# Other block widths, and another order of columns for each quarter of a block

## The chip, the cores and the metric

The kernel runs on one core of a Trainium2 chip. The metric is the device time of one execution in microseconds. The engines are TensorE (PE, with its weight loads shown apart as PEld), VectorE (DVE), ScalarE (ACT), GpSimd (POOL) and SyncE (SP), whose queue issues nearly all DMAs.

## What is computed

Two sequences of 6080 tokens with 256 channels pass through a gated scan along time, and each resulting token through a layer of 2048 hidden units with ELU. All is float32.

```python
    sig = 1.0 / (1.0 + np.exp(-f_logit))
    f = lower_bound[None, None, :] + (1.0 - lower_bound[None, None, :]) * sig
    i = 1.0 - f
    for t in range(S):
        h = f[:, t] * h + i[:, t] * x[:, t]
        y[:, t] = h
...
    h = x @ w_in
    g = np.where(h > 0.0, h, alpha * (np.exp(np.minimum(h, 0.0)) - 1.0))
    return (g @ w_out).astype(np.float32)
```

## The kernel before

Channels lie on the 128 partitions, tokens along the free dimension. The 6080 tokens of both sequences are worked on together, in 12 blocks along time: block 0 has `SHORT` = 448 tokens, blocks 1 to 11 have `TILE` = 512. `width(j)` and `tokens(j)` give a block's width and its place in memory.

Every operand of a matmul is split into a rounded part (`_hi`) and a rest (`_lo`), and a product is three matmuls: hi by hi, lo by hi, hi by lo. The layer's input product is computed in blocks 1 to 11 by seven products (`P1` to `P7`) for each pair of units instead of eight; there are 8 pairs (`q`) in a block. The function `product` issues its three matmuls at lines 866 to 868. The output product is `second`, with its three matmuls at lines 896 to 898. So a pair has 21 + 24 matmuls and a block 360, each of as many columns as the block has tokens. Block 0 is computed plainly: 32 tiles of 6 + 6 matmuls, 384 in all, at lines 968 to 1004 (input) and 896 to 898 (output); 17 of them are 512 columns wide although the block has 448. Ahead stand 18 matmuls on zeros in bfloat16 (line 1010) that warm the engine up.

Between the two products each tile passes through ScalarE (line 466 Relu of the negative, line 472 Exp, line 480 rounding to `g_hi`), VectorE (line 719, the ELU) and GpSimd (line 336, the rest `g_lo`). Beside that run, one block ahead, the gates (422, 613), the weighing (620), the scan (628) and the splitting of its result (451, 656, 356). The order on each engine is written out by hand as a function `whole(j, par)` for each engine, with semaphores between them. Blocks 3 to 10 are a hardware loop of two blocks a pass on PE, ACT and DVE; POOL and SP loop in a similar way. PE's instructions do not depend on a block's number except in the semaphore values they wait for.

The matmuls neither read nor write their columns in plain order. All three, moving operand in and result out, go through one function, so that each column still lands where it belongs:

```python
LINE = 8
APART = 4
...
def in_order(columns):

    return columns.rearrange("p (b a c) -> p a b c", a=APART, c=LINE)
```

The 512 columns are taken in runs of 8 neighbours; one run of every four is taken, 16 in all, and that is done in 4 passes over the columns. The pattern of a 512-column matmul is so 4 x 16 x 8, of a 448-column one 4 x 14 x 8.

Of the kernel before, what the change touches and what calls it, by code (L numbers as in the profile page):

```python
# [1 line left out]

# [19 lines left out]
SHORT = SEQ - (BLOCKS - 1) * TILE  # L22
# [8 lines left out]
LINE = 8  # L31
APART = 4
# [23 lines left out]
def in_order(columns):  # L56

    return columns.rearrange("p (b a c) -> p a b c", a=APART, c=LINE)


def width(j):
    return SHORT if isinstance(j, int) and j == 0 else TILE


def tokens(j):
    return bass.ds(0 if isinstance(j, int) and j == 0 else TILE * j - (TILE - SHORT), width(j))

# [8 lines left out]
def low_count(j, product):  # L76

    return j if product in (P6, P7, P3) else j + 1


def gated_scan_elu_ffn(nc, first_gate, forget_logit, value, w_in, w_out, out):
    ctx = ExitStack()
    with ctx:
# [139 lines left out]
        def _(sp):  # L223
# [24 lines left out]
            def reload(j):  # L248

                sp.wait_ge(carry_ready, BATCH * j)  # L250
                sp.wait_ge(a_lo_ready[P1], j)
                sp.wait_ge(sum_ready[1], j - 1)
                sp.wait_ge(sum_ready[2], j - 1)
                load_x(j, 0, 0)
                load_x(j, 1, 0)
                sp.wait_ge(a_lo_ready[P2], j)
                sp.wait_ge(sum_ready[3], j - 1)
                load_x(j, 0, 1)
                sp.wait_ge(a_lo_ready[P5], j)
                load_gate(j, 0, 0)  # L260
                sp.wait_ge(a_lo_ready[P6], j - 1)
                load_gate(j, 0, 1)
                sp.wait_ge(a_lo_ready[P7], j - 1)
                load_gate(j, 1, 0)
                sp.wait_ge(a_lo_ready[P3], j - 1)
                load_gate(j, 1, 1)

            def reload_last(j):
                sp.wait_ge(a_lo_ready[P4], j)
                load_x(j, 1, 1)  # L270
# [35 lines left out]
            with sp.Fori(2, BLOCKS - 3) as j:  # L306
                reload_last(j + 1)
                store(j - 1)
                reload(j + 2)
# [12 lines left out]
        def _(pool):  # L322
# [17 lines left out]
            def combine(j, k):  # L340
# [6 lines left out]
                if k == 1:  # L347
                    pool.wait_ge(sum_ready[0], j)
# [61 lines left out]
            with nc.Fori(0, (BLOCKS - 4) // 2, engines=(mybir.EngineType.Pool,),  # L410
                         hint_back_edge=True) as i:
                whole(2 * i + 2, 0)
                whole(2 * i + 3, 1)
# [4 lines left out]
        def _(act):  # L418
# [24 lines left out]
            def split(j, par, product):  # L443
# [5 lines left out]
                else:  # L449
                    act.wait_ge(sum_ready[(P5, P6, P7, P3).index(product)], j)  # L450
# [146 lines left out]
            with nc.Fori(1, (BLOCKS - 2) // 2, engines=(mybir.EngineType.Activation,),  # L597
                         hint_back_edge=True) as i:
                whole(2 * i + 1, 1)
                whole(2 * i + 2, 0)  # L600
# [8 lines left out]
        def _(dve):  # L609
# [22 lines left out]
            def combine(j, k):  # L632
# [6 lines left out]
                if k == 1:  # L639
                    dve.wait_ge(sum_ready[0], j)  # L640
# [6 lines left out]
                if k == 3:  # L647
                    dve.wait_ge(sum_ready[1], j)
# [198 lines left out]
            with nc.Fori(1, (BLOCKS - 2) // 2, engines=(mybir.EngineType.DVE,),  # L847
                         hint_back_edge=True) as i:
                whole(2 * i + 1, 1)
                whole(2 * i + 2, 0)  # L850
# [8 lines left out]
        def _(pe):  # L859
            def product(j, par, q, k, bank, start=False):  # L860
# [3 lines left out]
                into = in_order(bank[:, 0:w])  # L864
                a_h, a_l = in_order(a_h[:, 0:w]), in_order(a_l[:, 0:w])
# [161 lines left out]
            for t in range(TILES * (PAIRS - 1) - 1, TILES * PAIRS):  # L1027
                for half in range(HALVES):
                    second(j, t, half)
# [33 lines left out]
```

## Time and profile before

| | us |
|---|---|
| time before, two runs | 961.75 and 1004.33, median 983.04 |
| the profiled execution | 962.05 |
| its span in the profile | 960.2 |
| PE busy | 954.3 (99%) |
| ACT busy | 790.1 (82%) |
| DVE busy | 722.3 (75%) |
| POOL busy | 628.8 (65%) |

The span is the time between the first and the last instruction of the profile; 1.85 us of the execution lie around it. The profiled execution agrees with the faster of the two runs. A matmul's start is a measured time; its end is modelled, so that busy times of neighbouring matmuls overlap, and the distance from start to start is what tells how fast the engine goes.

### The profile page before, as it was taken

To read this page: it belongs to the slowest core of one execution; us is meant where nothing else is said; L and a number is where in the kernel's file an instruction comes from. 1 tells how busy PE (TensorE), PEld (TensorE's weight loads), DVE (VectorE), ACT (ScalarE), POOL (GpSimd) and SP (SyncE) were. 2 spreads that over 40 slices of the span, in tenths; PEclk is the share of its full clock that TensorE was granted. 3 is DMA by queue.
4 is the path that set the end of the run, shared out by engine and by line. 5 is a ranking of instruction groups with operands and counts; after the bars stand their busy time and mean duration, and the time that the engine had idled before them with its cause. 6 is when DMAs were issued, how large, how long until landed. Compare 5 with 4: busy or idle time off the path is not lost.

```text
span 960.2 us, 15016 instructions
## 1 busy us (share of the span) xinstructions
PE 954.3 (99%) x4362; PEld 815.4 (85%) x4362; DVE 722.3 (75%) x916; ACT 790.1 (82%) x1424; POOL 628.8 (65%) x477
## 2 busy tenths in 40 slices
PE   9999999999999999999999999999999999999998
PEld 6999888888888888888888888888888888888887
DVE  6998876976886796697688679679768867966444
ACT  7989888878888888888888888888888788887775
POOL 2578796576667668557656755856775765676544
PEclk9999999999999999999999999999999999999999
DMA  7212012002101201100210210120021021001001
GB/s 273 68 33 95 0 34 66 34 1 78 55 1 55 77 1 44 55 33 1 75 55 0 66 66 0 45 66 20 23 65 44 0 76 55 0 0 46 1 1 45
DMA packets 23078, 42.02 MB, mean 44 GB/s; under 512 B 2560, under 2 KB 4096, under 8 KB 23040
## 3 DMA queue, kind: packets, MB, share of 16 engines
q1 hardware_dynamic: 22752, 41.10, 13.2%
q10 hardware_dynamic: 288, 0.46, 0.1%
q8 instruction: 18, 0.29, 0.1%
q14 instruction: 20, 0.16, 0.1%
HBM read 29.10 MB, written 12.45 MB: 43 GB/s over the span
## 4 chain that ended last, share of the span: by engine, by line
PE 96%; ACT 2%; DVE 1%; issue 1%; POOL 0%; ACTq 0%; POOLq 0%
PE acc L896 17%; PE acc L898 17%; PE acc L897 17%; PE h L868 14%; PE h L866 14%; PE h L867 14%; ACT e L472 1%; PE h L1010 1%; PE h L1002 1%; PE h L1004 1%; PE h L1003 1%; ACT e L466 1%; DVE x L628 0%; PE h L968 0%; ACT w_out_hi L505 0%
## 5 line engine op out<-in xcount | busy, mean ns | idle before, releaser
L336 POOL TENSOR_TENSOR g_lo<-e,g_hi 128x512 fp32r<-128x512 f32 (+1 forms) x384 | 516.4, 1355 | 325.5 <-ACT g_hi L480 324.0
L466 ACT ACTIVATE e<-h 128x512 f32<-128x512 f32 (+1 forms) x379 | 224.8, 593 | 124.6 <-PE h L868 90.3
L719 DVE SCALAR_TENSOR_TENSOR e<-e,h 128x512 f32<-128x512 f32 (+1 forms) x379 | 256.8, 678 | 70.2 <-ACT e L472 69.1
L896 PE MATMUL acc<-g_hi,w_out_hi 128*128 128x512 f32 (+1 forms) x768 | 291.1, 379 | 0.4 <-DVE w_out_lo L690 0.4
L898 PE MATMUL acc<-g_hi,w_out_lo 128*128 128x512 f32 (+1 forms) x768 | 291.0, 379 | 0.0
L897 PE MATMUL acc<-g_lo,w_out_hi 128*128 128x512 f32 (+1 forms) x768 | 290.9, 379 | 0.0
L472 ACT ACTIVATE e<-e 128x512 f32<-128x512 f32 (+1 forms) x384 | 241.3, 628 | 9.7 <-issue 1.2
L480 ACT CAST g_hi<-e 128x512 fp32r<-128x512 f32 (+1 forms) x384 | 232.1, 604 | 19.3 <-DVE e L719 19.3
L866 PE MATMUL h<-a_hi,w_in_hi 128*128 128x512 f32 x616 | 234.7, 381 | 0.0
L868 PE MATMUL h<-a_hi,w_in_lo 128*128 128x512 f32 x616 | 234.7, 381 | 0.0
L867 PE MATMUL h<-a_lo,w_in_hi 128*128 128x512 f32 x616 | 234.7, 381 | 0.0
L896 PEld LDWEIGHTS acc<-g_hi,w_out_hi 128*128 128x128 f32 x768 | 143.9, 187 | 24.3 <-DVE w_out_lo L690 0.8
L897 PEld LDWEIGHTS acc<-g_lo,w_out_hi 128*128 128x128 f32 x768 | 143.9, 187 | 23.5
L898 PEld LDWEIGHTS acc<-g_hi,w_out_lo 128*128 128x128 f32 x768 | 143.9, 187 | 23.4
L868 PEld LDWEIGHTS h<-a_hi,w_in_lo 128*128 128x128 f32 x616 | 115.4, 187 | 20.1
L867 PEld LDWEIGHTS h<-a_lo,w_in_hi 128*128 128x128 f32 x616 | 115.4, 187 | 20.0
L866 PEld LDWEIGHTS h<-a_hi,w_in_hi 128*128 128x128 f32 x616 | 115.4, 187 | 20.0
L713 DVE TENSOR_TENSOR h<-p,h 128x512 f32<-128x512 f32 x88 | 60.9, 692 | 68.2 <-PE h L868 67.9
L628 DVE TENSOR_TENSOR_SCAN x<-opening,carry,x 128x512 f32<-128x512 f32 (+1 forms) x48 | 101.6, 2116 | 0.1
L698 DVE COPY p<-h 128x512 f32<-128x512 f32 x88 | 59.7, 679 | 43.4 <-PE h L868 42.9
L705 DVE TENSOR_TENSOR h<-p,h 128x512 f32<-128x512 f32 x88 | 60.7, 690 | 32.1 <-PE h L868 31.9
L620 DVE SCALAR_TENSOR_TENSOR x<-opening,x 128x512 f32<-128x512 f32 (+1 forms) x48 | 56.1, 1169 | 0.1
(77 smaller groups left out, 556.0 us busy)
## 6 DMA issues: line engine op xcount, KB each, us to landing
opening<-forget_logit SPq DMA_DIRECT2D x44, 256.0 KB, 2.7
x<-value SPq DMA_DIRECT2D x44, 256.0 KB, 2.7
out<-out_sb SPq DMA_DIRECT2D x44, 256.0 KB, 2.0
w_in_raw<-w_in SPq DMA_DIRECT2D x8, 256.0 KB, 5.4
w_out_raw<-w_out SPq DMA_DIRECT2D x8, 256.0 KB, 6.5
out<-out_sb SPq DMA_DIRECT2D x4, 224.0 KB, 1.9
x<-value SPq DMA_DIRECT2D x3, 224.0 KB, 6.1
opening<-forget_logit SPq DMA_DIRECT2D x2, 224.0 KB, 6.3
```

Source lines behind the costliest of these rows:

```text
L336: nc.gpsimd.tensor_tensor(g_lo[:, t % RING, 0:w], e[:, t % TILES, 0:w], g_hi[:, t % RING, 0:w].bitcast(F32), ALU.subtract).then_inc(g_lo_r ...
L466: nc.scalar.activation(e[:, i, 0:w], bank_of(j, t)[:, 0:w], ACT.Relu, scale=-1.0).then_inc(r_ready, 1)
L472: nc.scalar.activation(e[:, t % TILES, 0:w], e[:, t % TILES, 0:w], ACT.Exp, scale=-1.0).then_inc(e_ready, 1)
L480: nc.scalar.copy(g_hi[:, t % RING, 0:w], e[:, t % TILES, 0:w]).then_inc(g_hi_ready, 1)
L628: nc.vector.tensor_tensor_scan(x[:, b, i, 0:w], gate[:, b, i, 0:w], x[:, b, i, 0:w], carry[:, b, i], ALU.mult, ALU.subtract).then_inc(scan ...
L719: nc.vector.scalar_tensor_tensor(e[:, t % TILES, 0:w], e[:, t % TILES, 0:w], -1.0, bank_of(j, t)[:, 0:w], ALU.add, ALU.max).then_inc(g_rea ...
L866: nc.tensor.matmul(into, hi, a_h, start=start, stop=False, skip_group_check=True)
L867: nc.tensor.matmul(into, hi, a_l, start=False, stop=False, skip_group_check=True)
L868: return nc.tensor.matmul(into, lo, a_h, start=False, stop=True, skip_group_check=True)
L896: nc.tensor.matmul(bank, hi, g_h, start=opens, stop=False)
L897: nc.tensor.matmul(bank, hi, g_l, start=False, stop=False)
L898: done = nc.tensor.matmul(bank, lo, g_h, start=False, stop=closes)
```

## The change

The blocks become 496 and 504 tokens wide, then 512 and 504 in turns: six blocks of 504, five of 512 and one of 496 instead of eleven of 512 and one of 448. Since a block in a hardware loop now has a width by its parity, `width`, `tokens` and the semaphore counts go by a small class `Later` that holds the loop's number and whether it is odd; SP's loop takes two blocks a pass.

`in_order` takes a style. None is plain order, and block 0 has it. A style is (kind, groups, run, down): runs of `run` neighbours (4, 8 or 12 columns); kind T takes every `groups`-th run in `groups` passes as before; kind N with more than one group takes, within a stretch of groups times run columns, the runs one after the other, and N with one group takes all runs in a row; `down` walks a dimension backwards (1 the outer, 2 the middle, 4 the columns within a run). `STYLES` holds four for each of block 1, block 2, the odd blocks of the loop, its even blocks, and the last block: one for each quarter, which is two pairs. What was written as style (T, 4, 8, 0) in every block stands now in a part of the even blocks alone.

```diff
-SHORT = SEQ - (BLOCKS - 1) * TILE
+WIDTHS = (496, 504) + (512, 504) * (BLOCKS // 2 - 1)
+SHORT = WIDTHS[0]
...
-LINE = 8
-APART = 4
+T, N = range(2)
+FIRST_STYLE = None
+STYLES = (((T, 3, 8, 0), (T, 7, 8, 0), (T, 9, 8, 0), (T, 21, 8, 0)),
+          ((T, 2, 8, 0), (T, 4, 8, 1), (T, 4, 8, 2), (N, 1, 8, 2)),
+          ((T, 3, 12, 0), (T, 3, 4, 0), (T, 7, 4, 0), (T, 9, 4, 0)),
+          ((T, 4, 8, 0), (T, 4, 8, 4), (T, 8, 8, 0), (N, 4, 4, 2)),
+          ((T, 6, 4, 0), (T, 2, 12, 0), (T, 6, 12, 0), (T, 21, 4, 0)))
...
-def in_order(columns):
-
-    return columns.rearrange("p (b a c) -> p a b c", a=APART, c=LINE)
+def in_order(columns, style):
+    if style is None:
+        return columns
+    kind, groups, run, down = style
+    if kind == T:
+        steps = columns.rearrange("p (b a c) -> p a b c", a=groups, c=run)
+    elif groups == 1:
+        steps = columns.rearrange("p (o b c) -> p o b c", o=1, c=run)
+    else:
+        steps = columns.rearrange("p (b a c) -> p b a c", a=groups, c=run)
+    if down % 2:
+        steps = steps[:, ::-1]
+    if down // 2 % 2:
+        steps = steps[:, :, ::-1]
+    return steps[:, :, :, ::-1] if down // 4 else steps
...
 def width(j):
-    return SHORT if isinstance(j, int) and j == 0 else TILE
+    return WIDTHS[3 if j.odd else 2] if isinstance(j, Later) else WIDTHS[j]
...
             def whole(j, par, styles, before):
...
-                        second(j, TILES * at + i, half)
+                        second(j, TILES * at + i, half, styles[q // 2])
                     else:
-                        second(j - 1, TILES * (PAIRS + at) + i, half)
+                        second(j - 1, TILES * (PAIRS + at) + i, half, before)
```

No instruction moves against another on PE; the shapes change. The start of PE's program, before and then after (`h` and `acc` are banks of PSUM; a shape is partitions, then the pattern of columns from the outside in):

```order
L1010 MATMUL h<-e 128x512 x18
L968 MATMUL h<-a_hi,w_in_hi 128x4x16x8 x4
L968 MATMUL acc<-a_hi,w_in_hi 128x4x16x8 x2
L979 MATMUL h<-a_hi,w_plain_lo_54 128x4x16x8 x2
L983 MATMUL h<-a_lo,w_in_hi 128x4x16x8
L975 MATMUL h<-a_lo,w_in_hi 128x4x14x8
L979 MATMUL h<-a_hi,w_plain_lo_54 128x4x14x8 x2
```

```order
L1057 MATMUL h<-e 128x512 x18
L1015 MATMUL h<-a_hi,w_in_hi 128x512 x4
L1015 MATMUL acc<-a_hi,w_in_hi 128x512 x2
L1026 MATMUL h<-a_hi,w_plain_lo_54 128x512 x2
L1030 MATMUL h<-a_lo,w_in_hi 128x512
L1022 MATMUL h<-a_lo,w_in_hi 128x496
L1026 MATMUL h<-a_hi,w_plain_lo_54 128x496 x2
```

The wide ones stay 512 columns wide and the others grow from 448 to 496, all in plain order. In the loop on PE, where an odd block passes from its first quarter to its second, before and after:

```order
L898 MATMUL acc<-g_hi,w_out_lo 128x4x16x8
L952 REGISTER_ALU
L866 MATMUL h<-a_hi,w_in_hi 128x4x16x8
L867 MATMUL h<-a_lo,w_in_hi 128x4x16x8
L868 MATMUL h<-a_hi,w_in_lo 128x4x16x8
L922 REGISTER_ALU
L866 MATMUL h<-a_hi,w_in_hi 128x4x16x8
```

```order
L945 MATMUL acc<-g_hi,w_out_lo 128x3x14x12
L999 REGISTER_ALU
L913 MATMUL h<-a_hi,w_in_hi 128x3x14x12
L914 MATMUL h<-a_lo,w_in_hi 128x3x14x12
L915 MATMUL h<-a_hi,w_in_lo 128x3x14x12
L969 REGISTER_ALU
L913 MATMUL h<-a_hi,w_in_hi 128x3x42x4
```

The same instructions stand in the same places; the pattern and the width are other ones.

## Rows read from the trace of the kernel before

**Rows 1.** The page: span, busy time by engine, and the granted clock in 40 slices.

```profile
span 960.2 us, 15016 instructions
...
PE 954.3 (99%) x4362; PEld 815.4 (85%) x4362; DVE 722.3 (75%) x916; ACT 790.1 (82%) x1424; POOL 628.8 (65%) x477
...
PEclk9999999999999999999999999999999999999999
```

**Rows 2.** Waits between 80 and 955 us: engine, line, releaser, total us, times, longest.

```profile
POOL g_lo L336 <- ACT g_hi L480: 291.6, 236, 3.3
ACT e L466 <- PE h L868: 90.3, 167, 1.0
DVE h L713 <- PE h L868: 67.9, 68, 2.0
```

**Rows 3.** Timeline of PE: start us, duration us; the same place one block apart.

```profile
200.00 0.38 PE L897 MATMUL acc<-g_lo,w_out_hi 128*128 128x512 f32 x1
...
279.20 0.38 PE L897 MATMUL acc<-g_lo,w_out_hi 128*128 128x512 f32 x1
```

**Rows 4.** Timeline of PE: first matmul of block 1 and the last of all.

```profile
79.80 0.38 PE L866 MATMUL h<-a_hi,w_in_hi 128*128 128x512 f32 x1
...
956.58 0.40 PE L898 MATMUL acc<-g_hi,w_out_lo 128*128 128x512 f32 x1
```

**Rows 5.** Timeline of PE: a stretch of 169 matmuls of 448 columns, first and last.

```profile
12.49 0.35 PE L975 MATMUL h<-a_lo,w_in_hi 128*128 128x448 f32 x1
...
45.16 0.38 PE L1004 MATMUL h<-a_hi,w_plain_lo 128*128 128x448 f32 x1
```

**Rows 6.** Timeline of PE: warm-up matmuls after 6.2 us, merged where they overlap.

```profile
6.89 0.81 PE L1010 MATMUL h<-e 128*128 128x512 bf16 x3
...
7.32 0.38 PE L1010 MATMUL h<-e 128*128 128x512 bf16 x1
```

**Rows 7.** Timeline, from the first data to the first real matmul.

```profile
4.64 1.04 ACT L422 ACTIVATE opening<-opening 128x448 f32<-128x448 f32 x2 [1.69 <-DMA opening<-first_gate]
...
5.33 0.51 DVE L613 TENSOR_SCALAR opening<-opening,slope,offset 128x448 f32<-128x448 f32 x1 [0.45 <-ACT opening L422]
...
5.95 0.63 DVE L620 SCALAR_TENSOR_TENSOR x<-opening,x 128x448 f32<-128x448 f32 x1
...
6.61 1.15 DVE L628 TENSOR_TENSOR_SCAN x<-opening,carry,x 128x448 f32<-128x448 f32 x1
...
7.79 0.56 ACT L441 CAST a_hi<-x 128x448 fp32r<-128x448 f32 x1 [0.65 <-DVE x L628]
...
8.46 0.48 PE L968 MATMUL h<-a_hi,w_in_hi 128*128 128x512 f32 x1 [0.76 <-issue]
```

**Rows 8.** Timeline of PE: the last of four pauses in block 0.

```profile
66.28 0.38 PE L898 MATMUL acc<-g_hi,w_out_lo 128*128 128x448 f32 x1
66.79 0.45 PE L1002 MATMUL h<-a_hi,w_in_hi 128*128 128x448 f32 x1
67.07 0.37 PE L1003 MATMUL h<-a_lo,w_in_hi 128*128 128x448 f32 x1
67.28 0.36 PE L1004 MATMUL h<-a_hi,w_plain_lo 128*128 128x448 f32 x1
```

**Rows 9.** Groups by line and shape: x count | busy us, mean ns | idle us before.

```profile
L719 DVE SCALAR_TENSOR_TENSOR e<-e,h 128x512 f32<-128x512 f32 x352 | 240.2, 682 | 62.0 <-ACT e L472 61.3
...
L472 ACT ACTIVATE e<-e 128x512 f32<-128x512 f32 x352 | 222.6, 632 | 9.7 <-issue 1.2
...
L472 ACT ACTIVATE e<-e 128x448 f32<-128x448 f32 x32 | 18.6, 582 | 0.0
...
L719 DVE SCALAR_TENSOR_TENSOR e<-e,h 128x448 f32<-128x448 f32 x27 | 16.7, 617 | 8.2 <-ACT e L472 7.8
```

**Rows 10.** Timeline, the last copies and stores.

```profile
956.34 1.36 DVE L734 COPY out_sb<-acc 128x512 f32<-128x512 f32 x2 [1.29 <-PE acc L898]
...
957.06 1.00 SPq L276 DMA_DIRECT2D out<-out_sb  x2
```

**Rows 11.** DMA issues: KB each, median us to landing.

```profile
opening<-forget_logit SPq DMA_DIRECT2D x44, 256.0 KB, 2.7
...
opening<-first_gate SPq DMA_DIRECT2D x1, 225.0 KB, 3.9
```

More of the change, by code:

```diff
@@ L1 @@
 from contextlib import ExitStack
+from dataclasses import dataclass
 import concourse.bass as bass
@@ L53, with __add__, __sub__, __rmul__ @@
 PLACE = ((P1, P2), (P5, P4))
-def in_order(columns):
-    return columns.rearrange("p (b a c) -> p a b c", a=APART, c=LINE)
+def in_order(columns, style):
[13 more added lines that the diff above has]
+    return steps[:, :, :, ::-1] if down // 4 else steps
+@dataclass(frozen=True)
+class Later:
+    number: object
+    odd: bool
+    def __add__(self, k):
+        return Later(self.number + k, self.odd != bool(k % 2))
+    def __sub__(self, k):
+        return Later(self.number - k, self.odd != bool(k % 2))
+    def __rmul__(self, k):
+        return k * self.number
 def width(j):
-    return SHORT if isinstance(j, int) and j == 0 else TILE
+    return WIDTHS[3 if j.odd else 2] if isinstance(j, Later) else WIDTHS[j]
 def tokens(j):
-    return bass.ds(0 if isinstance(j, int) and j == 0 else TILE * j - (TILE - SHORT), width(j))
+    if not isinstance(j, Later):
+        return bass.ds(sum(WIDTHS[:j]), width(j))
+    known = 3 if j.odd else 2
+    step = (WIDTHS[2] + WIDTHS[3]) // 2
+    return bass.ds(step * j.number + (sum(WIDTHS[:known]) - step * known), width(j))
+def count(j):
+    return j.number if isinstance(j, Later) else j
 def split_count(j, product):
@@ L305, in _ @@
             reload(3)
[L306 to L309, printed above, removed]
+            reload_last(3)
+            store(1)
+            reload(4)
+            with sp.Fori(1, (BLOCKS - 4) // 2) as i:
+                for j in (Later(2 * i + 1, True), Later(2 * i + 2, False)):
+                    reload_last(j + 1)
+                    store(j - 1)
+                    reload(j + 2)
             reload_last(BLOCKS - 2)
@@ L859, in _, with product @@
         def _(pe):
-            def product(j, par, q, k, bank, start=False):
+            def product(j, par, q, k, bank, style, start=False):
                 w = width(j)
@@ L868, in product, with second @@
                 return nc.tensor.matmul(into, lo, a_h, start=False, stop=True, skip_group_check=True)
-            def second(j, t, half):
+            def second(j, t, half, style):
                 w = width(j)
@@ L902, in second, with whole @@
                     done.then_inc(acc_half, 1)
-            def whole(j, par):
+            def whole(j, par, styles, before):
                 def m(q, back, i, half):
@@ L922, in whole @@
                         pe.wait_ge(g_ready, TILES * (n - 2) + C21 + 1)
-                    product(j, par, q, P1, trunk(q), start=True).then_inc(p1_done, 1)
+                    product(j, par, q, P1, trunk(q), styles[q // 2], start=True).then_inc(p1_done, 1)
                     if q == 0:
@@ L926, in whole @@
                     pe.wait_ge(g_ready, TILES * (n - 1) + C12 + 1)
-                    product(j, par, q, P5, h[:, 2], start=True).then_inc(p5_done, 1)
+                    product(j, par, q, P5, h[:, 2], styles[q // 2], start=True).then_inc(p5_done, 1)
                     m(q, 2, C21, 0)
@@ L996, in first_product @@
                     hi, lo = plain_weights(unit, half)
-                    a_h, a_l = [in_order(part[:, 0:SHORT]) for part in a_parts(0, PLACE[b][half])]
+                    a_h, a_l = [in_order(part[:, 0:SHORT], FIRST_STYLE) for part in a_parts(0, PLACE[b][half])]
                     if t == TILES * PAIRS - 2 and half == 0:
-                        nc.tensor.matmul(in_order(h[:, 3]), hi, in_order(a_parts(0, P5)[0]), start=True, stop=False)
+                        nc.tensor.matmul(in_order(h[:, 3], FIRST_STYLE), hi, in_order(a_parts(0, P5)[0], FIRST_STYLE), start=True, stop=False)
                     else:
```

88 lines of the change are left out of this document (44 added, 44 removed).

## The prediction

> **What bounds the kernel now.** I read the page first [rows 1]: PE is busy 954.3 of 960.2 us, the next engine, ACT, 790.1, and the granted clock is in the top tenth in all 40 slices, the 2.4 GHz level of its two. Then the waits from 80 to 955 us [rows 2]: no row there has PE as the one that waits. Every other engine waits for PE or for an engine that does: ACT 90.3 us for line 868, DVE 67.9 us. So from block 1 on only PE's own rate counts, and the reader should look at the distance from start to start.
>
> From line 897 at 200.00 us to the same line 360 matmuls later it is 79.20 us, so 220.0 ns for each [rows 3]. From the first matmul of block 1 at 79.80 us to the last at 956.58 us [rows 4] there are 3989 steps, 30 of them still of block 0's 448 columns: 3959 x 0.2200 + 30 x 0.1933 = 876.8 us, and 876.78 us is what the rows say. PE does not lose one wait in 877 us. In block 0, 169 matmuls of 448 columns take 45.16 - 12.49 = 32.67 us, 193.3 ns each [rows 5].
>
> Two widths give a line: (220.0 - 193.3) / 64 = 0.417 ns per column, which is one column per cycle at 2.4 GHz, and what is left is 220.0 - 213.3 = 6.7 ns at 512 columns and 193.3 - 186.7 = 6.7 ns at 448. **So a matmul costs its columns plus 6.7 ns, 16 cycles**, whatever its operands are and whatever the other engines do. The only matmuls in plain order are the warm-up's. Three that follow each other start over 0.43 us [rows 6], 216 ns each, 4 ns less than the 220, but they read bfloat16 and load no float32 weights. The trace can't say whether the 4 ns are the order's or the type's. That is the open price of this change.
>
> **The widths.** With the constant of 6.7 ns, 504 columns cost 216.7 ns and 496 cost 213.3 ns. Six blocks of 360 matmuls go from 220.0 to 216.7: 2160 x -3.33 = -7.2 us. Five stay at 512. In block 0 the 17 wide matmuls stay, and 384 - 17 = 367 go from 193.3 to 213.3: +7.3 us. The sum is +0.1 us, since block 0 has 384 matmuls for a column and the others 360.
>
> **The start.** The chain to the first real matmul grows by 48 columns at each link: tanh, the gate (0.51 us), the weighing (0.63), the scan (1.15) and the rounding (0.56) [rows 7]. Exp takes 632 ns at 512 and 582 at 448 columns, the ELU 682 and 617 [rows 9], so 0.8 and 1.0 ns per column, some 40 and 50 ns for 48 columns; the scan by its own length 1.15 x 48 / 448 = 0.12 us. Together 0.3 us, and the first gate's transfer, 3.9 us for 225 KB [rows 11], adds up to 0.4 us if all of it goes by size and nothing if it is latency; a 256 KB load later lands in 2.7, so I take 0.1. The second scan and the rest of the second half stand behind the first on DVE and hold the next links: +0.4 us in all for the start, bounds 0.2 and 1.0.
>
> **The pauses in block 0.** PE pauses four times there, the last time at 66.28 us: 0.51 us to the next start and 0.28 to the one after, and then 0.21 us from 67.07 to 67.28 where 0.193 is the pace [rows 8]. Some 26 matmuls follow the pauses at about 0.20 to 0.21 us. A matmul of 496 columns takes 0.213 us anyway and hides this: -0.3 us. The pauses themselves I leave as they are, bounds -0.5 and +0.5, since the other engines grow by 8 to 9% in this block and PE by 10%.
>
> **From block 1 on.** What could take PE's cover away? At 504 columns PE is 1.5% faster, and the others are 8 columns shorter: 6 to 8 ns of 632 and 682, some 1.1%. PE gains at most 0.4% of 79 us = 0.3 us per block on them, and they wait for PE tens of times [rows 2]. Nothing. SP's loop is another one, but its loads land in 2.7 us [rows 11], and they are issued a block of 79 us ahead. Rows of 2016 instead of 2048 bytes change nothing that PE waits for. PE issues the same instructions in the same places, so no queue is lengthened.
>
> **The tail.** After the last matmul's start come two copies, 1.36 us, and the last stores [rows 10]: 8 columns less, -0.05 us.
>
> **The order of columns.** 3930 matmuls of blocks 1 to 11 have a pattern of runs. I take zero for each, because the nearest rows are those of the old pattern at two widths: 56 runs and 64 runs cost the same 6.7 ns, so a run costs nothing that can be seen. Block 0 in plain order I also take at zero; its lower bound is the warm-up's 216 ns: 384 x -4.0 = -1.5 us. The ends for all the others are in the rivals.
>
> The Trainium skill speaks against this change: "PSUM — Partial Sum Buffer", Specifications (TRN2), says of its 8-byte lines that any non-contiguous access pattern slows matmuls significantly, and "SBUF — State Buffer", Specifications (TRN2), that a 16-byte line wants at least two hits. By the trace the old pattern of 64 separate runs slows a matmul by at most 4 ns of 220 [rows 3, 6]; every new run is 4 columns or longer, thus fills whole lines, and the sum by that reading stays where it is.
>
> **The sum.** +7.3 - 7.2 + 0.4 - 0.3 - 0.05 = +0.2 us on the profiled execution's 962.05: **962.3 us**. It lies at the faster of the two runs shown, 961.75; the median of 983.04 is the mean of that and of 1004.33, which no row of the profile explains. I predict the level of the profiled execution; a measured median can hold a run like the second.
>
> **Rivals.**
>
> 1. *Each pass over the columns costs.* The 4 ns above the warm-up's pace could be those of the four passes, 1.0 ns each, and the rows don't exclude it, since both widths have four. The new styles make 1 to 9 passes, but 21 in 240 matmuls and 32 in the 510 of (N, 4, 4, 2). Over the 3930 matmuls they are 23,070 passes more than four each: +23.1 us, with block 0 in plain order -1.5 us: 984 us, 2.3% slower. It decides from 0.88 ns a pass up. For it: the only plain matmuls are the only faster ones. Against: the 4 ns can be all the type's.
>
> 2. *A short or a backward run is slow.* Patterns of 4 columns stand in 1890 matmuls and one in 360 walks backwards within the run, (T, 4, 8, 4). No row shows either. If the backward ones took two cycles a column, they would cost 360 x 213 ns = +77 us: 1039 us. By the smallest price, 4 ns spread over the 64 runs, 0.0625 ns for a run, the 108,600 additional runs cost +6.8 us, less 1.5 for block 0: 967.6 us. Against: the equal rest of 6.7 ns at 56 and 64 runs, where 8 runs at that price would be 0.5 ns.
>
> 3. *The orders save.* If none of the new orders has more than the warm-up's 2.7 ns, all 4344 matmuls gain 4.0 ns: -17.4 us, 945 us, 1.8% faster. This is the floor: a column per cycle stays. For it speaks only that some part of the 6.7 ns may be a meeting of one matmul's last lines with the next one's first.
>
> 4. *The second run's 1004 us come of the old order.* The profile that agrees with 961.75 shows full clock throughout, so the other 42 us are not in it. Should the old order bring them about and the new ones not, the time is the same 962, but 2.1% below the median of before. Nothing in the rows ties the two together.
>
> 5. *The change does not act*, the engine fetching columns in its own way whatever the pattern: the time is the forecast's, and only block 0's pace tells it.
>
> **Chances.** The forecast with its like (5, and all prices under a quarter of their ends) 0.62, the small price of 2 0.07, rival 3 in part or whole 0.05, rival 4 0.10, rival 1 0.10, the large price of 2 0.06. The range: the first three parts of the sum give 960 to 966; it goes up through 968 and 984, and on to 1003 since a run like the one at 1004.33 can enter a median; it goes down to 952, half of rival 3. That leaves out the large price of 2 and half of 3. About 2% is what a measurement of this kernel tells from no change. Faster by more: rival 4, 0.10. Slower by more: rival 1 and the large price, 0.16. Within: 0.74.
>
> **What the new profile would show.** Steps of 213.3 ns in block 0, 216.7 in the odd blocks and 220.0 in the even ones say the constant holds; 209 in block 0 says plain order saves 4 ns. If passes cost, the fourth quarter of the even blocks has steps of 248 ns and the last quarter of the last block 234. If backward runs are slow, the second quarter of the even blocks has them. The first `product` of block 1 should start at 79.8 + 7.3 - 0.6 (its 30 late matmuls of block 0) + 0.1 = 86.6 us. PE should still wait for nobody after that. The prediction is wrong if one quarter's step differs from the others of its width, or if PE waits for an engine from block 1 on.

## The result, and the profile after

The changed kernel takes 1048.38 us (1048.21 and 1048.56) against the kernel before's 983.04 (961.75 and 1004.33): 1.0895 times the time, 95% interval 1.0873 to 1.0917, against the faster of the two executions before; the other one has the time of a second, slower rate of the matmuls, which the experiments come to. It is slower by 87 us. The forecast was no change.

The page of the changed kernel, its span, its engines and its granted clock, beside [rows 1]:

```profile
span 1046.7 us, 14975 instructions
## 1 busy us (share of the span) xinstructions
PE 1040.4 (99%) x4362; PEld 822.9 (79%) x4362; DVE 725.9 (69%) x916; ACT 792.2 (76%) x1424; POOL 628.3 (60%) x477
...
PEclk9999999999999999999999999999999999999999
```

PE is as busy as before, 99%, the clock is at the 2.4 GHz level throughout, and DVE, ACT and POOL have the work they had. Only PE's own time has grown, by 86 us, for the same 4362 matmuls. The waits from 90 to 1040 us (engine, line, releaser, total us, times, longest) beside [rows 2]:

```profile
POOL g_lo L383 <- ACT g_hi L527: 377.7, 253, 5.1
ACT e L513 <- PE h L915: 171.7, 243, 1.7
DVE h L760 <- PE h L915: 94.2, 72, 3.0
```

Again everyone waits for PE and PE for nobody; ACT's wait has gone from 90.3 to 171.7 us. So each matmul is slower, and the timeline of PE says which. First and last of the 496-column matmuls ahead of block 1, the start of block 1, the start of the second and third quarter of an odd block of the loop, of the third and fourth quarter of the even block behind it, of the next block, and the last matmul (start us, duration us; the rows answer to [rows 3, 4]):

```profile
12.96 0.38 PE L1022 MATMUL h<-a_lo,w_in_hi 128*128 128x496 f32 x1
...
80.50 0.38 PE L945 MATMUL acc<-g_hi,w_out_lo 128*128 128x496 f32 x1
...
87.33 0.40 PE L913 MATMUL h<-a_hi,w_in_hi 128*128 128x504 f32 x1
...
276.53 0.39 PE L913 MATMUL h<-a_hi,w_in_hi 128*128 128x504 f32 x1
...
296.63 0.39 PE L913 MATMUL h<-a_hi,w_in_hi 128*128 128x504 f32 x1
...
380.51 0.39 PE L913 MATMUL h<-a_hi,w_in_hi 128*128 128x512 f32 x1
...
403.63 0.44 PE L913 MATMUL h<-a_hi,w_in_hi 128*128 128x512 f32 x1
...
427.63 0.40 PE L913 MATMUL h<-a_hi,w_in_hi 128*128 128x504 f32 x1
...
1042.76 0.40 PE L945 MATMUL acc<-g_hi,w_out_lo 128*128 128x504 f32 x1
```

Block 0, in plain order: from 12.96 to 80.50 us are 307 steps, 220.0 ns each, for 496 columns. From 276.53 to 296.63 is a quarter of 90 matmuls in the order (T, 3, 4, 0): 223.3 ns. From 380.51 to 403.63 is (T, 8, 8, 0): 23.12 us for 90, 256.9 ns. From 403.63 to 427.63 is (N, 4, 4, 2): 266.7 ns. From 87.33 to 1042.76 us the mean of 3989 steps is 239.5 ns, where it was 219.8. Most groups by order, over the whole trace (mean step in ns, and what it is above one column per 1/2.4 ns, in cycles of 2.4 GHz):

| order | columns | matmuls | ns | cycles above |
|---|---|---|---|---|
| plain | 496 | 367 | 220 | 32 |
| T 4 8 0, before | 512 | 3960 | 220.0 | 16 |
| T 3 4 0 | 504 | 360 | 223.3 | 32 |
| T 7 8 0 | 504 | 90 | 226.7 | 40 |
| T 4 8 0, after | 512 | 240 | 228.5 | 36 |
| T 3 12 0 | 504 | 240 | 230.8 | 50 |
| T 9 4 0 | 504 | 480 | 233.0 | 55 |
| T 7 4 0 | 504 | 360 | 233.3 | 56 |
| N 1 8 2 | 512 | 90 | 233.4 | 48 |
| T 4 8 4 | 512 | 360 | 235.7 | 54 |
| T 21 4 0 | 504 | 120 | 239.9 | 72 |
| T 21 8 0 | 504 | 120 | 241.7 | 76 |
| T 6 12 0 | 504 | 90 | 246.6 | 88 |
| T 8 8 0 | 512 | 360 | 256.9 | 105 |
| N 4 4 2 | 512 | 510 | 266.6 | 128 |
| T 6 4 0 | 504 | 60 | 286.5 | 183 |

Neither the number of runs nor that of passes sorts the table, nor does walking backwards. The old order itself has no longer one rate. At the start of each even block it stands in pieces of 6 or 9 matmuls between pieces of another order at 504 columns, and there its steps are 237 to 239 ns; the 33 matmuls from 352.01 us on, which nothing interrupts, have 220.7. The first such piece, six matmuls from line 913 on, and the next order behind it, 1.43 us for six:

```profile
338.62 0.39 PE L913 MATMUL h<-a_hi,w_in_hi 128*128 128x512 f32 x1
...
340.05 0.39 PE L943 MATMUL acc<-g_hi,w_out_hi 128*128 128x504 f32 x1
```

So a mean step belongs to an order in its surroundings. The weight loads are longer beside some of the slow matmuls. The groups of weight loads in the windows 352.1 to 358.5 us (old order), 380.6 to 403.5 (T 8 8 0) and 962.3 to 971.5 (T 6 4 0), x count, busy us and mean ns:

```profile
L943 PEld LDWEIGHTS acc<-g_hi,w_out_hi 128*128 128x128 f32 x6 | 1.1, 188 | 0.2
...
L944 PEld LDWEIGHTS acc<-g_lo,w_out_hi 128*128 128x128 f32 x16 | 3.1, 196 | 1.2
...
L943 PEld LDWEIGHTS acc<-g_hi,w_out_hi 128*128 128x128 f32 x6 | 1.2, 198 | 0.5
```

The loads are no measure of the matmuls: beside those of 266.6 ns they take 192 ns, and in the stretch of 256.9 ns those of line 945 take 188. Every matmul here brings its own 128 x 128 float32 weights, which are loaded beside the matmul ahead (PEld is busy for 822.9 us of the same span as PE's 1040.4). Two theories were made from this. **Theory R**: the reading of the moving operand out of SBUF meets the weight load that reads beside it, and which columns are read when decides how often. **Theory W**: the writing of the result into PSUM in an order sets the rate.

### The profile page after: what moved, and what is told of

Same layout as the page of the kernel before. It is cut to its first block, busy times and chain, and to the rows that moved or that the text cites. A ratio compares the mean times of both kernels' runs of the same rounds, so it can differ in the third digit from the quotient of the medians.

```text
span 1046.7 us, 14975 instructions
## 1 busy us (share of the span) xinstructions
PE 1040.4 (99%) x4362; PEld 822.9 (79%) x4362; DVE 725.9 (69%) x916; ACT 792.2 (76%) x1424; POOL 628.3 (60%) x477
## 4 chain that ended last, share of the span: by engine, by line
PE 99%; DVE 0%; DMA 0%; issue 0%; ACT 0%; DVEq 0%
PE acc L945 18%; PE acc L944 18%; PE acc L943 17%; PE h L915 14%; PE h L914 14%; PE h L913 14%; PE h L1050 1%; PE h L1051 1%; PE h L1049 1%; DMA opening<-first_gate 0%; PE h L1026 0%; DVE x L667 0%; DVE x L675 0%; PE acc L1051 0%; PE acc L1050 0%
## 5 line engine op out<-in xcount | busy, mean ns | idle before, releaser
L383 POOL TENSOR_TENSOR g_lo<-e,g_hi 128x504 fp32r<-128x504 f32 (+2 forms) x384 | 515.8, 1353 | 411.4 <-ACT g_hi L527 411.3
L513 ACT ACTIVATE e<-h 128x504 f32<-128x504 f32 (+2 forms) x379 | 225.0, 594 | 203.6 <-PE h L915 171.7
L945 PE MATMUL acc<-g_hi,w_out_lo 128*128 128x504 f32 (+2 forms) x768 | 309.9, 403 | 0.0
L944 PE MATMUL acc<-g_lo,w_out_hi 128*128 128x504 f32 (+2 forms) x768 | 308.8, 402 | 0.0
L943 PE MATMUL acc<-g_hi,w_out_hi 128*128 128x504 f32 (+2 forms) x768 | 308.2, 401 | 0.0
L766 DVE SCALAR_TENSOR_TENSOR e<-e,h 128x504 f32<-128x504 f32 (+2 forms) x379 | 256.5, 677 | 72.6 <-ACT e L519 72.2
L915 PE MATMUL h<-a_hi,w_in_lo 128*128 128x504 f32 (+1 forms) x616 | 248.6, 404 | 0.0
L519 ACT ACTIVATE e<-e 128x504 f32<-128x504 f32 (+2 forms) x384 | 241.4, 629 | 9.5 <-issue 1.1
L914 PE MATMUL h<-a_lo,w_in_hi 128*128 128x504 f32 (+1 forms) x616 | 247.7, 402 | 0.0
L913 PE MATMUL h<-a_hi,w_in_hi 128*128 128x504 f32 (+1 forms) x616 | 247.4, 402 | 0.0
L527 ACT CAST g_hi<-e 128x504 fp32r<-128x504 f32 (+2 forms) x384 | 232.2, 605 | 16.2 <-DVE e L766 15.6
```

The costliest lines, as they stand in the source:

```text
L383: nc.gpsimd.tensor_tensor(g_lo[:, t % RING, 0:w], e[:, t % TILES, 0:w], g_hi[:, t % RING, 0:w].bitcast(F32), ALU.subtract).then_inc(g_lo_r ...
L513: nc.scalar.activation(e[:, i, 0:w], bank_of(j, t)[:, 0:w], ACT.Relu, scale=-1.0).then_inc(r_ready, 1)
L519: nc.scalar.activation(e[:, t % TILES, 0:w], e[:, t % TILES, 0:w], ACT.Exp, scale=-1.0).then_inc(e_ready, 1)
L527: nc.scalar.copy(g_hi[:, t % RING, 0:w], e[:, t % TILES, 0:w]).then_inc(g_hi_ready, 1)
L766: nc.vector.scalar_tensor_tensor(e[:, t % TILES, 0:w], e[:, t % TILES, 0:w], -1.0, bank_of(j, t)[:, 0:w], ALU.add, ALU.max).then_inc(g_rea ...
L913: nc.tensor.matmul(into, hi, a_h, start=start, stop=False, skip_group_check=True)
```

## The experiments

Where no number of executions is given below, a kernel or scan was executed once.

**Orders with TensorE alone.** A kernel of matmuls only: 43 stretches of 60, every one with its own line, with the same layout of weights and moving operand as in the kernel (both at multiples of 512 bytes). The core of it:

```diff
+            def operands(name, w, read, write, shift, k):
+                at = P * (k % 8) + shift // 4
+                return (in_order(banks[:, (k // 3) % 8, 0:w], write), flat[:, at:at + P],
+                        in_order(moving[:, (k // 3) % 4, 0:w], read))
...
+            for k in range(EACH): last = nc.tensor.matmul(*operands('both_T4_512', 512, T4, T4, 0, k), **flags(k))
```

> TensorE alone: 43 stretches of 60 matmuls, each with the next weights loaded beside it, nothing else running and the results thrown away (the output is zeros). Both theories expect that the rates of the changed kernel come back here, with all other engines still: 220 ns in the old order at 512 columns, 227 ns in plain order at 512, 220 ns in plain order at 496, 257 for (T, 8, 8, 0), 267 for (N, 4, 4, 2), 286 for (T, 6, 4, 0). Theory R (the reading of the moving operand meets the weight load that runs beside it): reading in an order and writing plainly costs what both together cost, writing alone costs what plain order costs (227), a shift of the weights by 16 to 256 bytes changes the rate in the old order, and bfloat16, with half the bytes, is at 216 in every order. Theory W (the writing into PSUM sets the rate): the other way round, writing alone costs what both cost, reading alone 227, a shift of the weights changes nothing, and bfloat16 in the order (N, 4, 4, 2) is as slow as float32 in it. Rival 1 of the prediction, a price for each pass of the outer loop, expects 2 passes to be cheaper than 4 and 3 passes of 14 runs cheaper than 8 passes, and is nearly out already.

The timeline of PE, one row per stretch of 60 (start us, total us). The rows are: plain order at 512 columns; the old order at 512; the old order at 448; read in the old order and written plainly; read plainly and written in the old order; the start of the next; read in (N, 4, 4, 2) alone; written in (N, 4, 4, 2) alone; the start of the next; the old order with the weights shifted by 64 bytes; the start of the next; bfloat16 plain; bfloat16 in the old order; bfloat16 in (N, 4, 4, 2).

```profile
28.72 13.76 PE L149 MATMUL banks<-moving,weights 128*128 128x512 f32 x60
42.32 13.76 PE L151 MATMUL banks<-moving,weights 128*128 128x504 f32 x60
...
81.48 13.36 PE L157 MATMUL banks<-moving,weights 128*128 128x512 f32 x60
94.68 11.76 PE L159 MATMUL banks<-moving,weights 128*128 128x448 f32 x60
106.28 13.36 PE L161 MATMUL banks<-moving,weights 128*128 128x512 f32 x60
119.48 13.80 PE L163 MATMUL banks<-moving,weights 128*128 128x512 f32 x60
133.12 14.36 PE L165 MATMUL banks<-moving,weights 128*128 128x504 f32 x60
...
432.54 16.16 PE L207 MATMUL banks<-moving,weights 128*128 128x512 f32 x60
448.53 13.78 PE L209 MATMUL banks<-moving,weights 128*128 128x512 f32 x60
462.15 17.37 PE L211 MATMUL banks<-moving,weights 128*128 128x504 f32 x60
...
520.83 14.52 PE L219 MATMUL banks<-moving,weights 128*128 128x512 f32 x60
535.19 13.95 PE L221 MATMUL banks<-moving,weights 128*128 128x512 f32 x60
...
576.82 13.12 PE L227 MATMUL banks<-moving_b,weights_b 128*128 128x512 bf16 x60
589.78 13.11 PE L229 MATMUL banks<-moving_b,weights_b 128*128 128x512 bf16 x60
602.73 13.11 PE L231 MATMUL banks<-moving_b,weights_b 128*128 128x512 bf16 x60
```

Start to start over 60: plain 13.60 / 60 = 226.7 ns; the old order 13.20 / 60 = 220.0; reading in it alone 220.0, writing in it alone 227.3 with the first steps, 226.7 once it is steady. (N, 4, 4, 2) costs 266.5 when read and 227.0 when written. The old order at weights 64 bytes off costs 239.3. And bfloat16 runs at 215.8 to 216.0 ns in all three orders: that is what the warm-up's 216 ns [rows 6] were, the type's. The readings of theory R come in and those of theory W fail; only the shift by 256 bytes is no evidence, since its 230.8 ns turn out below to be a second rate of the old order. With all other engines still most of the changed kernel's rates come back within 1 ns, so those engines have no part in them. Five did not come exactly: (T, 8, 8, 0) had 241 ns instead of 257, (T, 21, 4, 0) 233.4 instead of 239.9, 496 columns in plain order 223.3 instead of 220.0, and (T, 3, 8, 0) and (T, 4, 8, 1) 236.6 and 236.3, each 3 ns above the kernel's.

**Plain order in the kernel before.**

```diff
-    return columns.rearrange("p (b a c) -> p a b c", a=APART, c=LINE)
+    return columns
```

> The kernel before with all columns in plain order. The changed kernel's block 0 in plain order takes 220.0 ns for 496 columns, 13.3 ns above one column per cycle, where the old order has 6.7. Both theories expect 13.3 ns on every matmul: 962.05 + 4344 x 6.67 ns = 991 us, the steps 226.7 ns at 512 columns and 200.0 at 448. The prediction as it stood expects 962 or, by the warm-up's pace, 945.

It took 989.51 us, the median of four executions, 1.0284 times (1.0262 to 1.0306), as the theories had it to 1.5 us; the old order is worth 28 us against plain order.

**One side at a time.** In the first kernel the moving operand is read in the old order and the result is written plainly, in the second the other way round. The two texts on record say it of each other's kernel; what ran is this, `apart` being the old order and `in_order` plain in the first, the names exchanged in the second:

```diff
                 into = in_order(bank[:, 0:w])
-                a_h, a_l = in_order(a_h[:, 0:w]), in_order(a_l[:, 0:w])
+                a_h, a_l = apart(a_h[:, 0:w]), apart(a_l[:, 0:w])
```

> The kernel before, with plain order for reading the moving operand, and the old order (T, 4, 8, 0) for writing the result alone; the columns of a result land in other places, so the output is not the reference's. Theory R: plain reading sets the rate, 991 us. Theory W: the old order of writing is what counts, 962 us.

> The kernel before, with the old order (T, 4, 8, 0) for reading the moving operand and plain order for writing the result; the columns of a result land in other places, so the output is not the reference's. Theory R: 962 us. Theory W: 991 us.

Read in the old order: 961.89 us. Written in it: 989.63. Read against the kernels themselves this is theory R, in both.

So as to have it once with a text that fits, and for the new orders, the same was done to the changed kernel, reading in its orders in one and writing in them in the other:

```diff
-                into = in_order(bank[:, 0:w], style)
+                into = bank[:, 0:w]
...
-                bank, g_h, g_l = in_order(bank, style), in_order(g_h, style), in_order(g_l, style)
+                bank, g_h, g_l = bank, in_order(g_h, style), in_order(g_l, style)
```

> The changed kernel with its orders for reading the moving operand, and plain order for writing the result; the columns of a result land in other places, so the output is not the reference's. Theory R: reading alone costs all of it, 1048 us. Theory W: plain writing, 998 us. (Of the two kernels before of this kind, the one called e2_read read in the old order and wrote plainly and e3_write read plainly and wrote in the old order, the other way round than their texts say; this one is described as it is.)

> The changed kernel with plain order for reading the moving operand and its new orders for writing the result; the columns of a result land in other places, so the output is not the reference's. Theory R: as with everything in plain order, 998.4 us. If writing costs anything of its own, more, up to 1048.

1048.70 us and 998.46 us. In the first, each order's mean step is that of the changed kernel to 0.1 ns. The writing of a result in any of these orders, all with runs of 4 columns or more, costs nothing that can be seen; the reading costs all.

**The widths alone.** The changed kernel with every style None:

```diff
-STYLES = (((T, 3, 8, 0), (T, 7, 8, 0), (T, 9, 8, 0), (T, 21, 8, 0)),
...
+STYLES = ((None,) * 4,) * 5
```

> The changed kernel's widths with all columns in plain order. By the rates in the traces so far, 226.7 ns at 512 and at 504 columns and 220.0 at 496: 3960 x 6.67 ns + 367 x 26.7 ns above the kernel before, so 962 + 26.4 + 9.8 = 998 us. By the sum of the prediction (16 cycles on every width) it would be 962. If the widths cost nothing against plain order at 448 and 512, it is 990.

998.40 us, against 989.51 for the old widths in plain order: the widths cost 8.9 us. In plain order 504 columns take 226.7 ns as 512 do, so the six narrower blocks give nothing back; and 448 columns took 202.7 ns, 496 take 220.0, so block 0 pays 367 x 17.3 ns = 6.4 us.

**More orders and distances.** The first scan's kernel with other cases, 36 matmuls in each.

> TensorE alone, 101 stretches of 36 matmuls (output zeros): many orders at 512 and 448 columns with weights and moving operand as they lie in the kernel, the old order and plain order with the weights shifted by 16 to 480 bytes. Theory R (reading the moving operand meets the weight load beside it in SBUF) expects the rate of one order to go up and down with the shift, between 216 and some 260 ns, and expects orders better than the old one's 220 ns to be possible down to bfloat16's 215.8. The rival (the pattern's own jumps cost, by their number and length) expects one rate per order whatever the shift, 220 for the old one and 227 for plain order; the first scan's five shifts of the old order already gave 227 to 240, so it is out unless those were after-effects of the stretch before.

No order at 512 columns beat 220.0 ns. The next was runs of 4 in 4 passes, 224.0; plain order and the orders that stay near it had 226.6 to 228.4, all others up to 278. Runs of 2 are another thing: rows are runs of 2 in 4 passes, then the old order with the weights 32 and 64 bytes off.

```profile
612.57 16.78 PE L293 MATMUL banks<-moving,weights 128*128 128x512 f32 x36
629.17 8.47 PE L295 MATMUL banks<-moving,weights 128*128 128x512 f32 x36
637.48 8.76 PE L297 MATMUL banks<-moving,weights 128*128 128x512 f32 x36
```

16.60 / 36 = 461 ns for a matmul. Here reading and writing both went by runs of 2, so which side costs it was not tested. The old order with the weights shifted by 32 to 480 bytes had 226.7 to 238.9 ns, and 220.0 at 256 bytes alone. But at no shift at all it had 230.6 here and 220.0 in the first scan, and in the first scan 230.8 at 256. So there are two rates. Plain order goes by the distance as well: 228.9 to 234.0 ns with the weights shifted by 16 to 448 bytes, but 227.2 at 256.

**Two rates for the old order.** 24 stretches of 48 in the old order, each after a pause of ScalarE's making:

```diff
+            pe.wait_ge(slept, 1)
             for k in range(EACH): last = nc.tensor.matmul(*operands('T4_0', 512, T4, T4, 0, k), **flags(k))
```

> TensorE alone (output zeros): 24 stretches of 48 matmuls in the old order at 512 columns, then 6 in plain order, 6 in (T, 8, 8, 0) and 4 of 448 columns in the old order, each stretch after a pause whose length grows by some ns from one to the next. If a stretch keeps the rate that it falls into at its start (as 496 columns in plain order had 220.0 ns in the changed kernel and 223.3 in the first scan), some of the 24 have another rate than 220 ns, perhaps around 230, which is what 1004 us for the kernel before would need on every matmul. If the rate goes by order and addresses alone, all 24 have 220.0 ns, and the 1004 us come from elsewhere.

Five of them on the timeline, alike in everything but the moment at which they begin:

```profile
97.71 11.34 PE L173 MATMUL banks<-moving,weights 128*128 128x512 f32 x48 [0.31 <-ACT pause L129]
109.37 11.34 PE L176 MATMUL banks<-moving,weights 128*128 128x512 f32 x48 [0.32 <-ACT pause L129]
121.03 10.84 PE L179 MATMUL banks<-moving,weights 128*128 128x512 f32 x48 [0.32 <-ACT pause L129]
132.19 11.34 PE L182 MATMUL banks<-moving,weights 128*128 128x512 f32 x48 [0.33 <-ACT pause L129]
143.86 11.34 PE L185 MATMUL banks<-moving,weights 128*128 128x512 f32 x48 [0.33 <-ACT pause L129]
```

Four of the 24 take 10.84 us, with steps of 219 and 221 ns from first to last. Twenty take 11.3 to 11.4, with steps of 227 to 237 ns, 230.7 in the mean. After their first steps none of these changes from one rate to the other. A rate is a pattern of steps that repeats: 219 and 221 ns in turns make 220.0, and 228, 229, 230, 230, 237 make 230.7. The old order at 448 columns has two as well, 193.3 ns in three stretches and 200.0 in the fourth. So has (T, 8, 8, 0), steps of 233 and 234 ns or of 246 to 277, and it can pass from one to the other: one of its six stretches was at 233 after four steps, one after 26 steps between 227 and 271, and four had not come to it within 48. The one in the first scan took about 28, which is why it had 241 ns and not 257. Plain order has one rate in six stretches.

Then in the kernel before, with one more wait on PE ahead of block 1:

```diff
                 second(0, TILES * PAIRS - LEAD, half)
+            pe.wait_ge(g_ready, TILES * PAIRS - 1)
             whole(1, 1)
```

> The kernel before with one more wait on TensorE ahead of block 1: it waits for the ELU of block 0's tile 30 (of 32), so that it stands for one to three microseconds and starts again at another moment. The last scan showed two rates for the old order at 512 columns, 220.0 ns in 4 of 24 stretches and 230.7 in 20, kept from the stretch's start to its end. If that holds in the kernel, where nothing stops TensorE from block 1 on, an execution takes either 963 to 965 us or 42 us more, 1005 to 1007, by chance or always the same one. If the rate goes by order and addresses alone, every execution takes 963 to 965.

Of its 11 executions one took 1004.66 us, one 965.23 and nine 961.4 to 961.9. Of the 13 of the kernel before on the same chip one took 1004.60, two 965.1 and 965.4 and ten 961.5 to 962.4. The wait cost nothing and changed nothing; the second time is the kernel's own. In the one execution with a trace PE did not even stop at it, so a start at another moment was not tested in the kernel. The executions at 965 us have no trace, and their 3 us stay open. The profiled execution was the one at 1004.66 us. The same line at the same place, 360 matmuls apart, beside [rows 3]:

```profile
200.18 0.40 PE L866 MATMUL h<-a_hi,w_in_hi 128*128 128x512 f32 x1
...
283.22 0.40 PE L866 MATMUL h<-a_hi,w_in_hi 128*128 128x512 f32 x1
```

83.04 / 360 = 230.7 ns, the second rate to the digit. It is so from 92 us to the end, for 3932 matmuls; 10.7 ns x 3960 = 42 us is what lies between 962 and 1004. By its time this is also the 1004.33 of the first table, of which no trace was kept. Full clock, no wait, the same matmuls.

It begins ahead of block 1 and of the added wait. In block 0 this execution comes back to 193.3 ns per matmul of 448 columns behind each of the first three pauses, as the kernel before does. Behind the fourth the kernel before is back at 193.3 after 16 uneven steps, and this one is at 200.0, the other rate of 448 columns: 18 steps in 3.60 us at the end of the block.

```profile
66.35 0.38 PE L898 MATMUL acc<-g_hi,w_out_lo 128*128 128x448 f32 x1
66.72 0.44 PE L1002 MATMUL h<-a_hi,w_in_hi 128*128 128x448 f32 x1
...
76.44 0.36 PE L1002 MATMUL h<-a_hi,w_in_hi 128*128 128x448 f32 x1
...
80.04 0.39 PE L866 MATMUL h<-a_hi,w_in_hi 128*128 128x512 f32 x1
```

The pause is 0.37 us from start to start here and 0.51 in [rows 8]. While widths alternate, up to 92 us, its 512-column steps lie anywhere from 219 to 238 ns; from about 94 us on the five steps of 230.7 ns repeat. That the length of the pause decides is not shown: it is one trace of each.

**Distance or place.** The moving operands 64 bytes further on, then all of SBUF's tiles 64 bytes further on, then the moving operands 256 bytes further on:

```diff
-        sb("room_of_edge", [P, P - EDGE])
+        sb("room_of_edge", [P, P - EDGE + 16])
...
-        sb("room_before", [P, -base % 512], mybir.dt.uint8)
+        sb("room_before", [P, -base % 512 + 64], mybir.dt.uint8)
...
-        sb("room_of_edge", [P, P - EDGE])
+        sb("room_of_edge", [P, P - EDGE + 64])
```

> The kernel before with all moving operands (and gates and x) 64 bytes further on in SBUF, the weights where they were. Theory R (the moving operand's reading meets the next weights' load, by the addresses of both): as weights shifted by -64 = 448 bytes in the scan, 229.9 ns at 512 columns, so 962 + 3960 x 9.9 ns and some more in block 0, about 1001 to 1005 us. Rival (the order's own jumps, addresses don't matter): 962.

> The kernel before with weights and moving operands both 64 bytes further on. If the distance between the two counts, 962 us (or 1004 by the second rate); if each one's own place counts, 1001 or more as with the moving operands alone.

> The kernel before with the moving operands 256 bytes further on and the weights where they were. Shifted by 64 bytes it took 988.5 us. The scans had the old order at 220.0 or 230.7 ns with the weights shifted by 256 bytes, as with no shift, and at neither with any other shift but one. If SBUF's lines come round again after 256 bytes: 962 us (or 1004 by the second rate). If only the same place within 512 bytes does: another time, 975 to 1010.

988.53, 961.81 and 961.96 us. The order is the same in all three and so is every instruction; what counts is the distance between weights and moving operand, and 256 bytes are as none. The 988.53 us are below the 1001 that the scan's 229.9 ns gave: in the kernel the steps were 231, 230 and 219 ns in turns, 226.7 in the mean. A distance has more than one rate, too, and a rate from a scan is not sure to be the kernel's.

**The weights' side.**

```diff
-                return (in_order(banks[:, (k // 3) % 8, 0:w], write), flat[:, at:at + P],
+                return (in_order(banks[:, (k // 3) % 8, 0:w], write), taken(k, at, step),
```

> TensorE alone (output zeros), two stretches of 36 matmuls for each pair of an order of the moving operand (18 of them) and a step between the weights' columns (1, 2 or 4 elements, weights interleaved with those of the next tiles). Theory R: the step changes the rate with the moving operand's order unchanged. A version faster than 220.0 ns would be worth a run in the kernel; down to bfloat16's 215.8 would be -18 us. If the moving operand's order alone makes the rate, the three steps have the same one.

The step changes the rate with the moving operand's order unchanged: plain order has 227.7 ns with adjacent weights, 233.3 with every second and 235 with every fourth; the old order 230, 231 and 238. The lowest of the 54 pairs was 223.5 ns once steady, runs of 4 in 4 passes with every second weight. No version faster than the kernel before was found, so none was run.

**Do the prices add up?** The changed kernel with the old order in the even blocks of the loop:

```diff
-          ((T, 4, 8, 0), (T, 4, 8, 4), (T, 8, 8, 0), (N, 4, 4, 2)),
+          ((T, 4, 8, 0), (T, 4, 8, 0), (T, 4, 8, 0), (T, 4, 8, 0)),
```

> The changed kernel with the old order (T, 4, 8, 0) in all four quarters of the loop's even blocks. If the price of an order is its own stretch's and adds up, it follows from the changed kernel's trace: 360 matmuls of (T, 8, 8, 0) from 256.9 to 220.0 ns, 510 of (N, 4, 4, 2) from 266.6 and 360 of (T, 4, 8, 4) from 236.0, together -42.8 us, 1006 us, since the first quarter of these blocks runs at 220.0 there; with the old order's second rate of 230.7 ns in all 1470 of them it is 1021. If the slow quarters are slow because orders change, or by something else than their order, less comes back.

1007.88 us, 2 us above the sum and far from 1021: these three orders in 1230 matmuls were worth 40.5 us. To about 2 us an order's price is its own stretch's. The expectation took 220.0 ns for the old order in these blocks; it has 222.2 over 1470 matmuls, because its pieces between other orders still take up to 239, and that is 3 us. The orders next to it moved as well, (T, 2, 12, 0) from 226.8 to 231.1.

**The sum of it.** From 961.7 us: plain order for the old one +27.8 (989.5), the widths +8.9 (998.4), the new orders against plain order +50.1 (1048.5). Of the 50, (N, 4, 4, 2) has 510 x 39.9 ns = 20.3 us and (T, 8, 8, 0) 360 x 30.2 ns = 10.9; the other orders share the rest.

## Why the prediction was wrong

- What bounds the kernel: right, before and after. PE goes at its own rate and waits for nobody.
- The widths: the step "a matmul costs its columns plus 6.7 ns, 16 cycles" failed. It was drawn from two widths, 448 and 512, in one order. It does not hold at 496 and 504 in plain order, where 32 and 40 cycles were above the columns. The +0.1 us forecast was +8.9, measured in plain order; in the kernel's own orders the widths were not measured apart.
- The order of columns: the step "I take zero for each" failed, and it carries nearly all of the miss: +27.8 for plain order and +50.1 for the new orders against it, 77.9 of 86.6 us. Its ground, equal rests at 56 and 64 runs, was a true reading, but of the wrong thing: it showed that the number of runs has no price and not that the order has none. What the runs showed in its place: the price goes by the order in which the moving operand is read, together with how the weights lie to it.
- The open 4 ns: I set plain order between 216 and 220 ns by the warm-up's rate. The warm-up's 216 ns are bfloat16's; float32 in plain order takes 226.7 ns at 512 columns. The old order was the cheap one, and block 0 lost 26.7 ns per matmul where I had put 20 for its width and at best -4 for the order. So the sentence that the old pattern slows a matmul by at most 4 ns was wrong too: against plain order it saves 6.7.
- Rival 1, a price for each pass, named the right direction and a wrong mechanism: 2 passes of 8 took 233 ns, 3 passes of 4 took 223, 6 passes of 4 took 286, 32 took 267. Rival 2's backward runs had 236 ns, not 427. Rival 3 is out, and so is rival 5, since every order had its own step.
- Rival 4, the 1004 us come of the old order: the tie that I did not see in the rows is there, the second rate of 230.7 ns. The chance I gave it, for a gain, was used up by the orders' price. Nor are the new orders free of it: (T, 8, 8, 0) has two rates in the scan, though the changed kernel's two executions lie 0.35 us apart.
- The start and the pauses: block 1 began at 87.33 us where 86.6 was said, and that this is near is luck, since two errors cancel. The start grew by 0.47 us (12.49 to 12.96), where 0.4 was said. The 338 matmuls from there to block 1 grew by 9.0 us instead of 6.8. The four pauses of block 0, which with their after-effects cost 1.9 us, were all gone where -0.3 was said: from 12.96 to 87.33 us the mean step is 220.0 ns.
- A count: blocks 1 to 11 have 3960 matmuls with a pattern, not 3930; the 23,070 passes are right for 3960.
- The sign that was given for being wrong, one quarter's step unlike the others of its width, came in; PE waited for nobody from block 1 on, as was said.
- The Trainium skill's line weighed in the prediction ("PSUM — Partial Sum Buffer", Specifications (TRN2), any non-contiguous pattern slows matmuls significantly) points the right way for the sum and not for the mechanism. Here plain order is slower than the old one, writing in orders costs nothing (998.46 against 998.40 us), and reading costs it all. What the Trainium skill's "SBUF — State Buffer", Specifications (TRN2), says, that a 16-byte line wants at least two hits, is met by runs of 2 columns, 8 bytes, too; yet with reading and writing in such runs a matmul took 461 ns, and which of the two costs it is open.

Shown: that the reading side makes the rate, that the distance to the weights within 256 bytes changes it, that the weights' own step changes it, that bfloat16 has one rate in three orders, and that one order at one distance has two rates. That the two reads get in each other's way at the same part of SBUF is argued from these; no run shows such a part. No kernel was run in which float32 matmuls stream without a weight load beside each, and that would be the direct test. The length of the weight loads speaks neither way: 188 ns beside 220.0 and beside 230.7, 192 beside 266.6, 198 beside 286.5. What makes a stretch fall into one of its rates stays open.

## What to carry to other kernels

Where float32 matmuls run back to back, each with its own weights, take the step from start to start for every shape and order in the trace, and price an order that no row shows from both sides by tens of nanoseconds, not by zero: two rows that agree in one order say nothing of another. Take an order's step from a stretch that nothing interrupts and from one that other orders interrupt; they can differ by 18 ns. Keep the distance between weight tiles and moving tiles a multiple of 256 bytes as it was measured, and measure again when a tile moves. When a kernel bound by one engine has two times some per cent apart at full clock, compare the steps of that engine in both before looking elsewhere.

## What the runs showed of the hardware that was not expected

- Float32 matmuls of 504 and 512 columns with a weight load beside each took 220.0 to 286 ns for reading orders with runs of 4 columns or more, and 461 ns for runs of 2 read and written; bfloat16 ones 215.8 to 216.0 ns in three orders.
- The order in which a result is written, in runs of 4 columns or more, made no difference that could be seen (998.46 against 998.40 us).
- The same matmuls at the same addresses held 220.0 or 230.7 ns each for some 900 us on end; the two traces part for good behind a pause in block 0, before matmuls of that width run alone. 1 of 13 executions of the kernel before took as long as the slower one.
- Matmuls can settle: (T, 8, 8, 0) had up to 28 uneven steps of 227 to 273 ns and then 233 and 234 without end, or did not come to it in 48.
- Plain order took 226.7 ns at 504 columns and at 512.
